# Fused attention, Fourier mixing and two MLPs: the loads and order of the first batch, and the order of the last step of phase 1

## The reference

```python
kv = einsum('bhsd,bhse->bhde', k, v); out = einsum('bhsd,bhde->bhse', q, kv)
x = out / sqrt(mean(out * out, -1) + 1e-06) * g_norm       # rms norm over a head's 64 features
u = x + real(fft(fft(x, axis=1), axis=2))                    # over 576 tokens, then 512 features
un = (u - mean(u)) / sqrt(var(u) + 1e-06)
x2 = u + relu(un @ w_ch1) @ w_ch2                            # 512 -> 2048 -> 512
u2 = x2 + ((x2^T @ U) @ V)^T                                 # rank 32, over the tokens
out = u2 + relu(u2 @ w_ch1') @ w_ch2'                        # second pair of weights
```

## Time and profile before

| | us |
|---|---|
| median of 3 runs | 1757.88 |
| lowest, highest | 1755.22, 1761.6 |
| the profiled execution | 1755.45 |
| its span | 1753.6 |
| TensorE busy in it | 1699.4 (97%) |
| VectorE busy | 1377.0 (79%) |
| ScalarE busy | 805.9 (46%) |
| GpSimd busy | 237.1 (14%) |

### The profile page before, as it was taken

One profiled execution on the slowest core, in us unless ns is written; L12 is line 12 of the kernel. 1 busy time (PEld: TensorE's weight loads), 2 busy tenths in 40 slices (PEclk: granted clock), 3 DMA queues, 4 the chain that ended last, 5 costly groups with the idle time before them and its releaser, 6 DMA issues.

```text
span 1753.6 us, 27424 instructions
## 1 busy us (share of the span) xinstructions
PE 1699.4 (97%) x10712; PEld 1645.8 (94%) x10712; DVE 1377.0 (79%) x1734; ACT 805.9 (46%) x1169; POOL 237.1 (14%) x171
## 2 busy tenths in 40 slices
PE   6999999899999999999999999999999999999999
PEld 5877789889999999999999999999999999999999
DVE  4999988988888887987976867956857758658567
ACT  1444555545445445445445445435434444443343
POOL 0474340020020020020110110100100100100200
PEclk8999999999999999999999999999999999999999
DMA  7677569998898898898886777966867767767663
GB/s 239 237 246 232 203 230 354 373 356 299 315 336 304 325 318 302 323 315 315 321 283 248 282 228 265 348 229 241 277 222 254 264 229 255 265 221 254 229 248 124
DMA packets 124321, 478.15 MB, mean 273 GB/s; under 512 B 13089, under 2 KB 47201, under 8 KB 83618
## 3 DMA queue, kind: packets, MB, share of 16 engines
q1 hardware_dynamic: 121762, 475.22, 77.3%
q10 hardware_dynamic: 2432, 1.18, 0.3%
HBM read 396.14 MB, written 78.64 MB: 271 GB/s over the span
## 4 chain that ended last, share of the span: by engine, by line
PE 75%; DVE 17%; issue 4%; ACT 1%; DMA 1%; SPq 1%; POOL 1%; DVEq 0%; ACTq 0%
PE pair L958 11%; PE pair L960 11%; PE pair L959 11%; PE pair L989 6%; PE pair L991 6%; PE pair L990 6%; PE pair L978 5%; PE pair L981 5%; PE pair L980 5%; DVE t_lo L1610 3%; DVE t_raw L1629 2%; PE pair L736 2%; DVE w_sb L1538 1%; PE tr_ps L846 1%; PE pair L757 1%
## 5 line engine op out<-in xcount | busy, mean ns | idle before, releaser
L958 PE MATMUL pair<-t_hi,w_sb 128*128 128x384 f32 x1344 | 461.4, 343 | 10.8 <-DVE h_sb L1647 7.2
L959 PE MATMUL pair<-t_lo,w_sb 128*128 128x384 f32 x1344 | 455.9, 339 | 0.0
L960 PE MATMUL pair<-t_hi,w_sb 128*128 128x384 f32 x1344 | 455.6, 339 | 0.0
L1291 ACT ACTIVATE t_hi<-t_raw 128x768 fp32r<-128x768 f32 x240 | 203.1, 847 | 280.0 <-DVE t_raw L1629 279.9
L1610 DVE TENSOR_TENSOR t_lo<-t_raw,t_hi 128x768 fp32r<-128x768 f32 x300 | 302.9, 1015 | 17.7 <-ACT t_hi L1279 16.4
L1856 POOL TENSOR_TENSOR t_raw<-a_sb 128x768 f32<-128x768 f32 x60 | 138.6, 2313 | 1267.0 <-PE pair L981 553.0
L978 PE MATMUL pair<-w_sb,t_hi 128*128 128x256 f32 x1008 | 285.4, 283 | 8.5 <-DVE t_lo L1610 7.9
L980 PE MATMUL pair<-w_sb,t_hi 128*128 128x256 f32 x1008 | 282.6, 280 | 0.0
L981 PE MATMUL pair<-w_sb,t_lo 128*128 128x256 f32 x1008 | 282.5, 280 | 0.0
L958 PEld LDWEIGHTS pair<-t_hi,w_sb 128*128 128x128 f32 x1344 | 252.8, 188 | 19.4 <-issue 14.9
L959 PEld LDWEIGHTS pair<-t_lo,w_sb 128*128 128x128 f32 x1344 | 253.0, 188 | 2.6
(11 more groups left out here) (187 smaller groups left out, 2218.7 us busy)
## 6 DMA issues: line engine op xcount, KB each, us to landing
w_sb<-wc SPq DMA_DIRECT2D x263, 1024.0 KB, 5.4
wc<-w_sb SPq DMA_DIRECT2D x25, 1024.0 KB, 6.3
w_raw<-wr1a SPq DMA_DIRECT2D x24, 512.0 KB, 6.6
w_raw<-wr1b SPq DMA_DIRECT2D x24, 512.0 KB, 4.0
w_raw<-wr2a SPq DMA_DIRECT2D x10, 1024.0 KB, 7.7
wc<-pb_v SPq DMA_DIRECT2D x16, 640.0 KB, 7.0
u_dram<-x_sb SPq DMA_DIRECT2D x24, 384.0 KB, 5.5
res_sb<-u_dram SPq DMA_DIRECT2D x36, 256.0 KB, 7.4
```

The source lines that it names most:

```text
L958: nc.tensor.matmul(ps, w_hi, hi[:, x, :], start=(fresh and x == 0), stop=False, skip_group_check=True)
L959: nc.tensor.matmul(ps, w_hi, lo[:, x, :], start=False, stop=False, skip_group_check=True)
L960: last = nc.tensor.matmul(ps, w_lo, hi[:, x, :], start=False, stop=(x == 1), skip_group_check=True)
L1291: nc.scalar.activation(t_hi[r][:, :, :], t_raw[r][:, :, :], ACT.Copy).then_inc(hi_ready, 1)
```

## The change

Four things. k and v of batch 0 are loaded by blocks of tokens, whole rows of 2048 bytes, five pieces each, and the products of batch 0 run over the pieces in that order. The four transform constants go on ScalarE's queue, two behind its first copy of kv, two behind its first root; the identity goes behind the two weight units on SyncE's; each set has its own semaphore. Group 2 of batch 0 goes ahead of `kv_products(1)`, and on VectorE its sum and normalisation ahead of the first fold. In the last step of phase 1 the copies, the square of group 2 and the first cosine copy go ahead of the sums of `more_sb`, and `unfold(6, 0)` and `unfold(6, 1)` go between the folds of batch 7; GpSimd adds the first tile of batch 6 ahead of the sum of slot 1, and the other two ahead of `raw(0, 0)`.

```diff
--- before.py
+++ after.py
@@ -339,9 +339,9 @@
         def sem(name):
             return ctx.enter_context(nc.semaphore(name))
 
-        const_loaded = sem("const_loaded")
+        const_loaded, feat_loaded, eye_loaded = sem("const_loaded"), sem("feat_loaded"), sem("eye_loaded")
         gn_loaded = sem("gn_loaded")
-        kv0_loaded, q0_loaded = [[sem(f"{what}0_loaded{n}") for n in range(m)] for what, m in (("kv", NP), ("q", NT))]
+        kv0_loaded, q0_loaded = [[sem(f"{what}0_loaded{n}") for n in range(m)] for what, m in (("kv", 5), ("q", NT))]
         kv_loaded, q_loaded = [[sem(f"{what}_loaded_{r}") for r in range(2)] for what in ("kv", "q")]
         kv_zeroed, warm_zeroed = sem("kv_zeroed"), sem("warm_zeroed")
         kv_summed, kv_copied = sem("kv_summed"), sem("kv_copied")
@@ -490,23 +490,18 @@
                 sp.dma_start(wc2[1][i - 1, h].rearrange("p l f c -> p (l f c)"),
                              job_sb[:, :, :, :, :].rearrange("p l f x c -> p (l f x c)").bitcast(F32)).then_inc(job_stored, 16)
 
-            for n in range(NP):
-                cols = slice(128 * n, 128 * (n + 1))
-                sp.dma_start(k_sb[0][:, 0:4, cols], k_main[0][:, :, cols]).then_inc(kv0_loaded[n], 16)
-                sp.dma_start(k_sb[0][0:64, 4, cols], k_rest[0][:, cols]).then_inc(kv0_loaded[n], 16)
+            for t in range(4):
+                sp.dma_start(k_sb[0][:, t, :], k_main[0][:, t, :]).then_inc(kv0_loaded[t], 16)
+            sp.dma_start(k_sb[0][0:64, 4, :], k_rest[0]).then_inc(kv0_loaded[4], 16)
             q0 = q_t[0].rearrange("p h (g n) -> p h g n", g=NT)
             for g in range(NT):
                 sp.dma_start(q_sb[0][:, :, 2 * PT * g:2 * PT * (g + 1)], q0[:, :, g]).then_inc(q0_loaded[g], 16)
             sp.dma_start(gn_sb[:, :], g_norm.partition_broadcast(PT)).then_inc(gn_loaded, 16)
             load_kv(1)
             load_q(1)
-            sp.dma_start(cseq_sb[:, :, :], c_seq).then_inc(const_loaded, 16)
-            sp.dma_start(sseq_sb[:, :, :], s_seq).then_inc(const_loaded, 16)
-            sp.dma_start(cft_sb[:, :, :], c_feat).then_inc(const_loaded, 16)
-            sp.dma_start(sft_sb[:, :, :], s_feat).then_inc(const_loaded, 16)
-            sp.dma_start(ident[:, :], eye).then_inc(const_loaded, 16)
             load_unit(UNITS[0])
             load_unit(UNITS[1])
+            sp.dma_start(ident[:, :], eye).then_inc(eye_loaded, 16)
 
             def store_u(b):
                 for g in range(NT):
@@ -722,14 +717,22 @@
 
         @block.tensor
         def _(pe):
+            def first_kv_products():
+
+                for t in range(5):
+                    pe.wait_ge(kv0_loaded[t], 32)
+                    rows = 128 if t < 4 else 64
+                    for h in range(NP):
+                        cols = slice(128 * h, 128 * (h + 1))
+                        last = nc.tensor.matmul(kv_ps[:, cols], k_sb[0][0:rows, t, cols], v_sb[0][0:rows, t, cols],
+                                                start=(t == 0 and h == 0), stop=(t == 4), skip_group_check=True)
+                last.then_inc(kv_summed, 1)
+
             def kv_products(b):
                 r = b % 2
-                if b:
-                    pe.wait_ge(kv_loaded[r], 64 * ((b + 1) // 2))
-                    pe.wait_ge(kv_copied, 2 * b)
+                pe.wait_ge(kv_loaded[r], 64 * ((b + 1) // 2))
+                pe.wait_ge(kv_copied, 2 * b)
                 for h in range(NP):
-                    if b == 0:
-                        pe.wait_ge(kv0_loaded[h], 64)
                     cols = slice(128 * h, 128 * (h + 1))
                     for t in range(5):
                         rows = 128 if t < 4 else 64
@@ -766,7 +769,7 @@
             def seq_transform(b, first):
                 pe.wait_ge(folded, NT * (b + 1))
                 if first:
-                    pe.wait_ge(const_loaded, 80)
+                    pe.wait_ge(const_loaded, 32)
                 for s in range(4):
                     seq_slot_free(b, s, first)
                     ps, dt = seq_ps[s % 2], s % 2
@@ -807,6 +810,8 @@
                     last.then_inc(seq_done, 1)
 
             def feature_transform(b, first, more=True, tiles=range(NT)):
+                if first:
+                    pe.wait_ge(feat_loaded, 32)
                 for t in tiles:
                     s = 5 + t
                     m = PT + 1 if t == 0 else PT
@@ -834,10 +839,9 @@
                     kv_products(b + 1)
                 feature_transform(b - 1, first)
 
-            kv_products(0)
-            attention(0, (0, 1), True)
+            first_kv_products()
+            attention(0, (0, 1, 2), True)
             kv_products(1)
-            attention(0, (2,), True)
             for b in range(1, B):
                 phase1_step(b, b == 1, b < B - 1)
 
@@ -1003,6 +1007,7 @@
             for s in range(3):
                 last_seq_part(s, 0)
             pe.wait_ge(scaled, 6 * B)
+            pe.wait_ge(eye_loaded, 16)
             for q in range(4):
                 first_turn(q)
             pe.wait_ge(folded, NT * (B - 1) + 2)
@@ -1193,17 +1198,9 @@
                     copy_seq(b - 1, (1,))
                     root(b, 1)
                     copy_seq(b - 1, (2,))
-                if not more:
-                    ln_total(4)
                 copy_seq(b - 1, (3,))
-                if not more:
-                    ln_total(5)
                 copy_g(b - 1)
                 copy_row(b)
-                if not more:
-                    ln_centre(slice(4, 6), 1)
-                    ln_square(4)
-                    ln_square(5)
                 square(b, 2, False)
                 if more:
                     root(b, 2)
@@ -1211,10 +1208,15 @@
                     copy_cos(b - 1, 0, first)
                     copy_cos(b - 1, 1, first)
                 else:
+                    copy_cos(b - 1, 0, first)
+                    ln_total(4)
+                    ln_total(5)
+                    root(b, 2)
+                    copy_cos(b - 1, 1, first)
+                    ln_centre(slice(4, 6), 1)
+                    ln_square(4)
+                    ln_square(5)
                     ln_root()
-                    copy_cos(b - 1, 0, first)
-                    copy_cos(b - 1, 1, first)
-                    root(b, 2)
                 copy_cos(b - 1, 2, first)
                 for n in SUMMED.get(b, ()):
                     split_unit_hi(UNITS[n])
@@ -1222,23 +1224,26 @@
                     for q in range(4):
                         ln_total(q)
 
-            for n in range(NP):
-                cols = slice(128 * n, 128 * (n + 1))
-                act.dma_start(v_sb[0][:, 0:4, cols], v_main[0][:, :, cols]).then_inc(kv0_loaded[n], 16)
-                act.dma_start(v_sb[0][0:64, 4, cols], v_rest[0][:, cols]).then_inc(kv0_loaded[n], 16)
+            for t in range(4):
+                act.dma_start(v_sb[0][:, t, :], v_main[0][:, t, :]).then_inc(kv0_loaded[t], 16)
+            act.dma_start(v_sb[0][0:64, 4, :], v_rest[0]).then_inc(kv0_loaded[4], 16)
             act.wait_ge(warm_zeroed, 1)
             nc.scalar.activation(warm_sb[:, 1:2], warm_sb[:, 0:1], ACT.Sqrt)
             act.wait_ge(kv_zeroed, 1)
             copy_kv(0, first=True)
+            act.dma_start(cseq_sb[:, :, :], c_seq).then_inc(const_loaded, 16)
+            act.dma_start(sseq_sb[:, :, :], s_seq).then_inc(const_loaded, 16)
             act.wait_ge(eps_set, 1)
             square(0, 0, True)
             square(0, 1, True)
             root(0, 0)
+            act.dma_start(cft_sb[:, :, :], c_feat).then_inc(feat_loaded, 16)
+            act.dma_start(sft_sb[:, :, :], s_feat).then_inc(feat_loaded, 16)
             root(0, 1)
+            square(0, 2, True)
             copy_row(0)
+            root(0, 2)
             copy_kv(1)
-            square(0, 2, True)
-            root(0, 2)
             def deviation(n):
                 act.wait_ge(var_eps, n - 2)
                 nc.scalar.activation(sd_sb[:, :], ve_sb[:, :], ACT.Sqrt).then_inc(sd_ready, 1)
@@ -1544,9 +1549,9 @@
                 normalise(b, 0)
                 normalise(b, 1)
                 fold(b, 0, False)
+                sums(b, 2)
                 if not more:
-                    ln_scale()
-                sums(b, 2)
+                    unfold(b - 1, 0, first)
                 normalise(b, 2)
                 if more:
                     fold_tokens(b, 1, False)
@@ -1555,10 +1560,10 @@
                     unfold(b - 1, 1, first)
                     fold(b, 2, False)
                 else:
+                    ln_scale()
                     fold(b, 1, False)
+                    unfold(b - 1, 1, first)
                     fold(b, 2, False)
-                    unfold(b - 1, 0, first)
-                    unfold(b - 1, 1, first)
                 unfold(b - 1, 2, first)
                 fix_row(b - 1)
                 for n in SUMMED.get(b, ()):
@@ -1568,9 +1573,9 @@
             normalise(0, 0)
             sums(0, 1)
```

(10 more changed lines are left out.)

## The result

| | before | after |
|---|---|---|
| median, same chip (9 runs each) | 1756.79 us | 1764.22 us |
| ratio after / before | | 1.0038, 95% interval 1.0025 to 1.0052 |
| span of the profiled execution | 1753.6 us | 1762.3 us |
| first transform starts | 45.60 | 51.82 |
| second transform | 69.65 | 78.38 |

The kernel became slower by 7.4 us. 1748.7 was forecast, range 1743 to 1754. The loss is made in the first 78 us and then carried: the last step starts 8.73 us late, exactly as late as the second transform.

A forecast was written before the change was run, and what follows sets the result against it. Mostly TensorE matmul work, untouched; saturated VectorE steps carry time won at the start to their end. Start 5.0 plus end 2.6, 1.1 and 0.5 gave 9.2 us: 1748.7 us forecast, range 1743 to 1754.

The forecast's parts named there:

- (1): Start, batch 0 by token rows: first copy at 10.7 instead of 14.15, 3.5 us earlier (bounds 1.2 and 4.5).
- (3): Start, group 2 before batch 1: VectorE's 7.00 us idle goes; first transform near 40.7, whole start gains 5.0 us.
- (2): Start, constants on ScalarE's queue: s_seq's issue holds ScalarE 5 us at the long end; c_seq lands between 35 and 41.
- D: Rival, start: ScalarE held as SyncE was, 12.38 us plus 2.24; folds end at 47.4, total 1755.4; chance 0.07.
- B: Rival, start: no hold on ScalarE, its queue being empty; folds end at 34.9, total about 1745.5; chance 0.25.
- (4): Last step of phase 1, reordered ScalarE work: waits go, first turned chunk copied at 217.5 instead of 220.11, 2.6 us.
- (5): End, GpSimd adds batch 6 earlier: VectorE's w_sb split takes 1.21 instead of 3.71 us; gains 1.1 and some 0.5 us.
- E: Rival, slower: feature issues stand until c_seq is gone; folds 6 to 12 us late, 1766 at far end; chance 0.05.

The follow-up runs named there:

- e3: The changed kernel with the old last step of phase 1, so only the start is changed: 1761.75 us, ratio 1.0019.
- e6: The changed kernel with c_seq split, then whole c_seq and s_seq loaded again, unneeded, on ScalarE's queue to hold it: 1765.0 us, ratio 1.0031 to 1.0064.
- e5: The changed kernel with c_seq issued last of the four constants, so nothing of ScalarE's stands behind it: 1768.51 us, ratio 1.0048 to 1.0073.
- e1: The changed kernel with c_seq loaded as 96 and 1 partitions, still on ScalarE's queue: 1750.76 us, ratio 0.9954.
- e7: e1 with the sum of weight slot 1 moved from GpSimd to VectorE: 1750.85 us, ratio 0.9945 to 0.9973.
- e9: The changed kernel with c_seq split and the old last step of phase 1: 1751.77 us, ratio 0.9963 to 0.9986.
- e11: The changed kernel with c_seq split and all four constants back on SyncE's queue: 1751.81 us, ratio 0.9969.
- e12: e1's kernel run again (c_seq split, rows, new last step): 1751.30 us, ratio 0.9968.
- e13: e9's kernel run again (c_seq split, rows, old last step): 1750.94 us, ratio 0.9957 to 0.9980.
- e17: e13's kernel run again, beside e16 on the same chip: 1751.56 us, ratio 0.9973.
- e16: The kernel before with only batch 0's loads and products by token rows: 1755.56 us, ratio 1.0005.
- e15: The changed kernel with c_seq split, batch 0 by column blocks and the old last step: 1756.92 us, ratio 1.0001.
- e8: The kernel before with only c_seq split into 96 and 1 partitions, on SyncE's queue: 1757.41 us, ratio 0.9994.
- e4: The kernel before with only the last step of phase 1 in the new order: 1756.22 us, ratio 0.9986.
- e14: e10's kernel run again (c_seq split, column blocks, new last step): 1755.56 us, ratio 0.9996.
- e10: e1 with batch 0 loaded and multiplied by column blocks, as in the kernel before: 1756.05 us, ratio 0.9992.

## Why the prediction was wrong, step by step

**(1) Rows.** The first copy was forecast at 10.7; it came at 14.09 in the profile of after and at 13.0 in the mean of 13. The gain of 2.5 us is inside the bounds given (1.2 to 4.5); the place was wrong by 2.3 us. That the edit needs (3) to be worth anything, and (3) needs it, was not seen: the prediction added them as terms of a sum.

**(2) Constants on ScalarE's queue.** This is the step that failed, in two terms. The trace's packets show both. Packets of 3468 bytes begun in each 2 us from 14 us on; 97 are c_seq's, one engine's work, and 96 s_seq's, which make the peak:

```
from        14 16 18 20 22 24 26 28 30 32 34 36 38 40 42 44 46 48 50
before       0  0  0  0  0  7 48 66 13 13 13 14 11  8  0  0  0  0  0
after        0  0  3  4  7  3  4 35 61 17  8  8  6  8  9  9  5  4  2
```

The hold was foreseen as a kind, from the earlier trace rows; its size was not. I took 12 rows at 0.45 us, 5 us at most. It was 12.31, 12.30 and 14.50 us (after, e3, e6), near the 12.38 us of the earlier trace rows. The first row of c_seq goes only 4.3 us after its issue, when SyncE's packets of the same engine are out of the way; then it is 2 rows a us, as taken (a row takes 0.14 us there, an 8 KB packet of the other queue 0.31 to 0.43); but 19 rows are gone when ScalarE is let go (21 in e3), not 12. So the nearest row of the trace was the better price, and the rival that used it (D) stood at 0.07. That the two agree to 0.1 us is luck: in before 10.8 us of the hold had passed when c_seq's first row started, in after 3.8.

The landing did more harm. I let c_seq land at 35 to 41; it landed at 51. Its rows go at 7 a us in before, in after at 2, then 4 and at the end 2 a us again, for 32 us. The prediction charged 287 KB of other work on that engine, 10.3 us, and at the far end batch 2's 147 KB. But SyncE, rid of the constants, had work for the engine all the time: it issued batch 2's load at 25.5 instead of 36.95 and a further one from 41.6. From c_seq's issue to its last row the trace has 10.6 MB of other packets, an estimated 660 KB for each of 16 engines; in before it was 5.3 MB. The Trainium skill, "DMA: Bandwidth & Descriptors", section "Queues, rings and completion order", says that an engine takes turns among its queues packet by packet; 0.14 and 0.31 to 0.43 us in turn are the 2 rows a us of the first stretch, so the trace agrees. e5 shows this term by itself. No rival had a landing that alone decides.

**(3) Group 2 ahead.** Right as a mechanism: no idle time before group 2's sum in any kernel that has it. The forecast first transform, 40.7, is near what the kernels show where (2) is put right (39.2 to 40.8 in e1, e7, e9, e11, e12, e13 and e17), but by luck, since these have no hold. Without one the prediction had the folds end at 34.9 (B). The first copy came 2.5 us later than taken, and the folds of e1 lose another 2.4 us beside GpSimd's sums of pb_raw (L1465, L1476 to L1478: 1.21, 0.87, 0.69 and 0.92 us where 0.68, 0.42, 0.15 and 0.42 are usual, and 1.03 for 0.69 at L1463), which in before ran behind them, from 45.39. The prediction had charged nothing for that. The gain of 5.0 us is there in the profiles (45.60 to 40.05 in e1) and, with the rows, in the medians (e17 against e16, which also differ in the place of the constants: 4.0 us).

**(4) The last step.** The waits went as forecast: ScalarE's sums of more_sb ran without one and TensorE's 2.23 us were gone. What took their place was VectorE's block by GpSimd, 4.39 us for 1.28 of work, or 2.09 for 0.17. The prediction had charged 0.6 us for the adds beside the folds and nothing for the sum of slot 1. That sum hardly moved (215.00 before, 215.3 in the clock of the last step after); the multiplication did, from 216.68 to 213.8, so that it meets the adds and all of the sum, and the norm's shift now stands behind it instead of ahead. The prediction named the right rule for it in step (5), and didn't apply it one step earlier. The first turned chunk was to be 2.6 us earlier and was 0.5 later.

**(5) The split of w_sb** came at 1.21 us and the stall behind it is gone, both as forecast. But the 3.71 us were no mark of the old order: with the old end it took 1.21 or 1.22 us in five profiles (e3, e9, e15, e16, e17), 2.17 in e8 and 4.22 in e13. The old end has its waits in phase 2 either way (1.5 and 1.9 us in those five). With (4) the end was to be worth 4.2 us; the medians say -0.4, 1.4 (e12 to e15), 2.5 (e4) and -3 (after against e3). e7 took most of the block away; whether its 1.8 us at the first matmul of phase 2 reach the time, six runs can't tell.

**The sum** of 9.2 us would have been 8.1 or 5.6 us by e1's and e12's ratios (0.9954, 0.9968), had c_seq been split. The range missed since its slow end was built from D and E at small chances; E had the right sign, but its point, a hold of 15 us, was too high (e6, held for 14.50 us, is 0.5% slower), and after got there through the landing.

**Left open:** why group 2 ahead in column blocks shows nothing in two medians (e14, e15) though the profiles have the last step 0.6 us earlier (e14), 4.1 earlier (e10) and 2.9 later (e15). These profiles differ more than the effect, with their first copy; that of the kernel before, 14.15, is the earliest of the six with columns, so the profile that all are held against is a favourable one.

## What to carry to other kernels

The load of 97 partitions ran on one DMA engine, at 28 GB/s; with the other queue's packets on that engine it took 32 us instead of 16, and an issue behind it on the same queue stood 12 us. Split it (96 and 1), and never put it in front of an engine that computes; when a hold is in the trace already, take its own duration as the price ahead of a model of it.

Two edits at the start of a pipeline need not add up: rows alone and group 2 ahead alone showed nothing, both together 0.3%. Ask of each what it is worth without the other, and which wait then ends last. And work moved to an idle GpSimd should be asked which VectorE instruction it will then stand beside.

## What the hardware showed that was not expected

- A held issue on a queue that was empty but for c_seq: 12.31 and 12.30 us in after and e3, let go when 19 and 21 of the 97 packets on the one engine had begun. In e6, with other loads ahead, it was 14.50 us and 12 packets, on SyncE's queue in before 12.38 us and 12 packets. The same two loads with c_seq as 96 and 1 partitions: 0.35, 0.54 and 0.32 us.
- With c_seq split, SyncE's issue of the identity, behind the two weight units, still stands 12.79 us (e17) and 13.29 (e1). So a queue holds its issuer without any one-engine load too, when enough is outstanding. It cost nothing here, as the next load of SyncE's was early enough.
- VectorE beside GpSimd: 2.09 us instead of 0.17 for six columns, 4.39 instead of 1.28 for two normalisations. The Trainium skill, "SBUF — State Buffer", section "Who interferes with whom", says that the port pair the two share is an exclusive lock, and that issue order decides who blocks; the small instruction that waits out the large one agrees.
- The landing of the first loads has a spread that a single profile hides: the first copy came at 12.42 to 14.09 us with rows, at 14.15 to 16.71 with columns.
